# Attention with values stationary in two column groups, probabilities scaled on GpSimd, and partitions moved by SBUF transfers

## The reference

```
q, k, v: (2, 8, 768, 64), proj: (64, 6)
bucket(q), bucket(k): six sign bits of q @ proj and k @ proj
scores = where(bucket(q) == bucket(k), q @ k.T / 8, -1e9)
attn = exp(scores - rowmax); attn = attn / (rowsum + 1e-9)
x = attn @ v                                  -> (1536, 512)
h = x @ w_in (512, 2048); g = P(h) / Q(h);    x2 = g @ w_out
route: expert = argmax(x2 @ w_gate); out = gate * relu(x2 @ w1[e]) @ w2[e], 8 experts
```

## Time and profile before

| | us |
|---|---|
| median of 3 runs | 906.86 |
| lowest, highest | 903.77, 913.84 |
| the profiled execution | 908.51 |
| its span | 906.7 |
| busy PE / DVE / ACT / POOL | 853.0 / 761.4 / 598.5 / 365.1 |
| chain that ended last: PE, DVE, ACT | 72%, 15%, 5% |
| granted TensorE clock, mean | 0.98 |

### The profile page before, as it was taken

The page is one execution under the profiler, slowest core; times in us unless marked ns, Lnnn a source line. Parts: engine busy times, 40 slices in busy tenths (PEclk is TensorE's granted clock), DMA queues, the critical chain, the costliest instruction groups (busy, mean ns, idle before and its releaser), DMA issues.

```text
span 906.7 us, 17000 instructions
## 1 busy us (share of the span) xinstructions
PE 853.0 (94%) x5056; PEld 751.2 (83%) x5056; DVE 761.4 (84%) x1364; ACT 598.5 (66%) x1106; POOL 365.1 (40%) x321
## 2 busy tenths in 40 slices
PE   5999999999999998888999999999789999999996
PEld 3788989889898897777999998997678888888885
DVE  4789888888988759999877877876789999999992
ACT  1565666556566457567766776765279888998883
POOL 2553333534334406564222222222134666666542
PEclk7999999999999899999999999999989999999999
DMA  4111111211110101111000000002478111344950
GB/s 94 36 49 40 47 38 38 55 43 53 38 38 20 44 2 47 58 47 47 2 1 12 23 0 11 24 0 104 150 270 285 61 38 43 130 130 139 341 186 0
DMA packets 57472, 63.05 MB, mean 70 GB/s; under 512 B 29347, under 2 KB 39587, under 8 KB 57444
## 3 DMA queue, kind: packets, MB, share of 16 engines
q1 hardware_dynamic: 54404, 54.57, 19.2%
q0 software_dynamic: 3040, 8.13, 2.8%
HBM read 102.53 MB, written 8.13 MB: 122 GB/s over the span
## 4 chain that ended last, share of the span: by engine, by line
PE 72%; DVE 15%; ACT 5%; issue 4%; DMA 2%; POOL 1%; DVEq 0%; ACTq 0%; SPq 0%; POOLq 0%
PE ps_s L513 11%; PE ps_t L678 11%; PE ps_s L655 11%; PE ps_o L429 10%; PE ps_t L531 7%; PE ps_t L418 6%; PE ps_o L531 3%; PE ps_s L404 3%; PE ps_s L406 3%; DVE inv_b L1046 3%; DVE k_mask L909 2%; DVE row_max L923 2%; DVE num_b L1044 2%; PE ps_s L664 2%; PE ps_p L393 2%
## 5 line engine op out<-in xcount | busy, mean ns | idle before, releaser
L429 PEld LDWEIGHTS ps_o<-v_raw,probsT 128*128 128x128 f32 x1152 | 142.8, 194 | 5.7 <-issue 5.6
L1325 POOL TENSOR_TENSOR g_lo<-num_b,g_hi 128x384 fp32r<-128x384 f32 x64 | 65.3, 1020 | 190.2 <-ACT g_hi L793 113.4
L429 PE MATMUL ps_o<-v_raw,probsT 128*128 128x64 f32 x1152 | 141.5, 273 | 0.2 <-ACT x_pair L733 0.2
L1208 DVE TENSOR_TENSOR w_lo<-w_raw,w_hi 128x1024 fp32r<-128x1024 f32 x76 | 125.6, 1709 | 2.9 <-ACT w_hi L840 0.9
L719 ACT ACTIVATE probs<-ps_s,exp_bias,exp_scale 128x768 f32<-128x768 f32 x96 | 94.9, 989 | 44.5 <-DVE exp_bias L933 44.5
L923 DVE TENSOR_REDUCE row_max<-ps_s 128x1 f32<-128x768 f32 x96 | 91.1, 949 | 16.3 <-PE ps_s L406 16.3
L418 PE MATMUL ps_t<-ident,probs 128*128 128x128 f32 x576 | 82.4, 280 | 8.8 <-DVE probsT L938 6.6
L733 ACT ACTIVATE x_pair<-ps_o,row_inv 128x64 f32<-128x64 f32 x96 | 30.1, 314 | 88.5 <-PE ps_o L429 88.5
L513 PE MATMUL ps_s<-xT_hi,win_hi 128*128 (+1 forms) x256 | 88.0, 344 | 0.0
L513 PE MATMUL ps_s<-xT_hi,win_lo 128*128 (+1 forms) x256 | 86.2, 337 | 0.0
L418 PEld LDWEIGHTS ps_t<-ident,probs 128*128 128x128 f32 x576 | 66.1, 146 | 24.3 <-issue 20.5
(11 more groups left out here) (210 smaller groups left out, 2271.9 us busy)
## 6 DMA issues: line engine op xcount, KB each, us to landing
w_raw<-in_moe_w_dram SPq DMA_DIRECT2D x152, 512.0 KB
win_raw<-in_moe_w_in_dram SPq DMA_DIRECT2D x16, 256.0 KB, 2.8
x_sb<-in_moe_w_out_dram SPq DMA_DIRECT2D x16, 256.0 KB, 2.6
qk_raw<-in_q_dram SPq DMA_DIRECT2D x16, 192.0 KB, 3.1
qk_raw<-in_k_dram SPq DMA_DIRECT2D x16, 192.0 KB, 3.4
v_raw<-in_v_dram SPq DMA_DIRECT2D x16, 192.0 KB, 2.4
mlp_out_scratch<-x_sb SPq DMA_DIRECT2D x12, 256.0 KB, 2.0
out_dram<-y_sb,idx_scatter POOLq DMA_INDIRECT x19, 2.8
```

What stands on the lines that cost most here:

```text
L429: mm = pe.matmul(ps_o[:, 0:D], probsT[slot][:, t, :], v_raw[par][:, t, :], start=(t == 0), stop=(t == QT - 1))
L1208: dve.tensor_tensor(w1_lo[par][:, c, :], w1_raw[:, c, :], w1_hi[par][:, c, :].bitcast(F32), ALU.subtract).then_inc(w1_lo_made, 1)
```

## The change

On PE, `attend` now takes two tiles at once, every second step: v (64 columns) is stationary and the turned probabilities (128 columns) move. One tile's result goes to PSUM partitions 0 to 63, the other's to 64 to 127 (two column groups of the array). x so comes out turned, and `turn_x` is gone. The two halves of a hash go to two column groups as well; `hash_w` is 64 columns wide.

The probabilities are scaled before they are turned, by POOL (`normalise`); ACT's `norm` is gone. DVE makes the inverses of two tiles together. There are three buffers of probabilities and four of turned ones. PE turns a tile two steps after its exp and attends four steps after; scores are made two steps ahead.

High parts of q and k, masks and x go through staging tiles, and SP moves them to their places by transfers from SBUF to SBUF: four for the high parts, four for the masks, four for x, per head. One `mask_rows` per head replaces four. POOL's w_in split uses a one-input instruction. At the start q and k of both heads are turned before the first hash; at the end the first three `mlp_up` are put between the last steps, and the second stage waits for the transfers of x.

```diff
@@ SP
+            def place_hi(par):
+                hi = qkT_hi[:].bitcast(F32)
+                for target, rows, part in ((k_mask, slice(0, D), slice(D, P)), (q_mask, slice(0, D), slice(0, D)),
+                                           (k_cross, slice(0, D), slice(D, P)), (q_cross, slice(D, P), slice(0, D))):
+                    sp.dma_start(target[par][rows, :].bitcast(F32), hi[part, :]).then_inc(hi_in[par], 16)
+            def place_masks(par):
+                for hb in range(2):
+                    cols = slice(hb * HALF, (hb + 1) * HALF)
+                    for target, row in ((q_mask, HC * hb), (k_mask, HC * hb + ZK)):
+                        sp.dma_start(target[par][D:KR, cols].bitcast(F32),
+                                     mask_st[row:row + MR, :]).then_inc(mask_in[par], 16)
+            def place_x(i, par):
+                for parts, target in ((x_hi_st, xT_hi), (x_lo_st, xT_lo)):
...
+                    for g in range(2):
+                        sp.dma_start(blocks[:, where, g, :, :], parts[par][g * D:(g + 1) * D, :].bitcast(F32).rearrange(
+                            "p (o b n) -> p o b n", o=1, b=BLOCKS)).then_inc(x_out[par], 16)
+            def attention_head(i, par, first=False, more=True, more_qk=True):
+                m = 2 * i + par
+                if not (first and par == 0):
+                    if more or par == 0:
+                        hold(sp, masked, m + 2)
+                        hold(sp, scored, QT * m)
+                        place_masks(1 - par)
+                        hold(sp, attended, BLOCKS * m)
+                        load_v(m + 1, 1 - par)
+                    hold(sp, x_lo_made, START + m)
+                    place_x(i if par else i - 1, 1 - par)
+                if more:
+                    hold(sp, win_lo_made, m + 1)
+                    load_win(m + 2, par)
+                    if more_qk:
+                        hold(sp, qk_turned, 2 * m + 6)
+                        load_qk(m + 4, par)
+                    hold(sp, qk_hi_made, m + 3)
+                    hold(sp, scored, QT * (m + 1))
+                    place_hi(par)
@@ PE
+            def hash_qk(i, par):
+                pe.wait_ge(qk_copied, 4 * i + 2 * par + 2)
+                for hb in range(2):
+                    mm = pe.matmul(ps_p[HC * hb:HC * (hb + 1), 0:HALF], hash_w[:],
+                                   qkT[:, hb * HALF:(hb + 1) * HALF], start=True, stop=True)
             def scores(...)
+                    pe.wait_ge(mask_in[par], 64 * (i + 1))
+                    pe.wait_ge(hi_in[par], 64 * (i + 1))
+                    pe.wait_ge(qk_parts, 4 * i + 2 * par + 2)
+                if not first:
+                    pe.wait_ge(exped, STEPS * i + c - 1)
             def turn_probs(...)
-                pe.wait_ge(exped, n + 1)
+                pe.wait_ge(normed, n + 1)
+            def attend(i, c):
+                n, par, b = STEPS * i + c, c // QT, (c % QT) // 2
+                pe.wait_ge(pT_lo_half, n + 2)
+                pe.wait_ge(pT_hi_half, n + 2)
+                if b == 0:
+                    pe.wait_ge(v_in[par], 16 * (i + 1))
+                    pe.wait_ge(x_lo_made, START + 2 * i + par)
                 for t in range(QT):
-                    mm = pe.matmul(ps_o[:, 0:D], probsT[slot][:, t, :], v_raw[par][:, t, :],
-                                   start=(t == 0), stop=(t == QT - 1))
+                    for g in range(2):
+                        mm = pe.matmul(ps_o[g * D:(g + 1) * D, b * P:(b + 1) * P], v_raw[par][:, t, :],
+                                       probsT[(c + g) % 4][:, t, :], start=(t == 0), stop=(t == QT - 1))
+            def step(i, c):
+                if c % 2 == 0 and there(i, c - 4):
+                    attend(*at(i, c - 4))
+                if there(i, c - 2):
+                    turn_probs(*at(i, c - 2), first=isinstance(i, int) and STEPS * i + c == 2)
+                if there(i, c + 2):
+                    scores(*at(i, c + 2))
+                if there(i + 1, 0):
+                    if c % QT in (1, 3):
+                        turn_qk(i + 1, c // QT, c % QT // 2)
+                    if c % QT == 5:
+                        hash_qk(i + 1, c // QT)
@@ ACT
+            def step(i, c):
+                if there(i, c):
+                    exp_scores(i, c)
+                if c % QT in (2, 4) and there(i + 1, 0):
+                    copy_qk(i + 1, c // QT, c % QT // 2 - 1)
+                if c % QT == 3 and there(i, c - QT):
+                    x_hi(*((i, 0) if c >= QT else (i - 1, 1)))
+                if there(i, c - 2):
+                    copy_probs(*at(i, c - 2))
@@ DVE
+            def mask_rows(i, par, first=False):
...
+                dve.tensor_scalar(mask_st[:], ps_p[:, 0:HALF], hash_thr[:, 2:3], hash_thr[:, 3:4],
+                                  ALU.is_ge, ALU.mult).then_inc(masked, 1)
+            def step(i, c):
+                if there(i, c + 1):
+                    find_max(*at(i, c + 1))
+                    row_scale(*at(i, c + 1))
+                    row_bias(*at(i, c + 1))
+                if c % 2 == 1 and there(i, c):
+                    invert_sums(i, c)
+                if there(i, c - 2):
+                    copy_probs(*at(i, c - 2))
+                if c % QT == 0:
+                    if c == 0 and there(i, 0) and not (isinstance(i, int) and i == 0):
+                        mask_rows(i, 1)
+                    if c == QT and there(i + 1, 0):
+                        mask_rows(i + 1, 0)
+                if c % QT == 3 and there(i, c - QT):
+                    x_lo(*((i, 0) if c >= QT else (i - 1, 1)))
@@ POOL
+            def normalise(i, c):
+                slot = probs[c % 3]
+                if c % 2 == 0:
+                    pool.wait_ge(inverted, PAIR_TILES * i + c // 2 + 1)
+                pool.tensor_scalar(slot[:], slot[:], row_inv[:, c:c + 1], None, ALU.mult).then_inc(normed, 1)
+            def attention_pair(i, more):
+                for par in range(2):
+                    for j in range(QT):
+                        normalise(i, QT * par + j)
+                        if j == 1:
+                            split_win(i, par)
+                        if more and j == 3:
+                            hi_of_qk(i + 1, par)
+                            lo_of_q(i + 1, par)
+                        if more and j == 5:
+                            lo_of_k(i + 1, par, STEPS * i + QT * (par + 1))
@@ PE, between attention and the second stage
+            step(PAIRS, 0)
             pe.wait_ge(win_lo_made, PIECES)
...
             mlp_up(0, 0)
+            step(PAIRS, 1)
+            mlp_up(0, 1)
+            step(PAIRS, 2)
+            pe.wait_ge(exped, STEPS * PAIRS)
+            mlp_up(0, 2)
+            pe.wait_ge(x_lo_made, START + HEADS)
+            for par in range(2):
+                pe.wait_ge(x_out[par], 16 * START + 64 * PAIRS)
```

More of the change, by code:

```diff
@@ L482, in _ @@
             pe.wait_ge(ident_made, 2)
-            for hb in range(2):
-                turn_qk(0, 0, hb, first=True, bank=(ps_p, ps_t[0])[hb])
+            turn_qk(0, 0, 0)
+            turn_qk(0, 0, 1, bank=ps_t[0])
+            turn_qk(0, 1, 0, bank=ps_t[1])
+            turn_qk(0, 1, 1, bank=ps_s[0][:, 0, :])
+            pe.wait_ge(hash_made, 7)
+            hash_qk(0, 0)
             pe.wait_ge(consts_in, 64)
@@ L487, in _ @@
             pe.matmul(ps_o[:, 0:6], ones_row[:], ab_row[:, 0:6], start=True, stop=True).then_inc(coef_ps, 1)
[L488 to L504 removed]
+            pe.wait_ge(qk_copied, 4)
+            scores(0, 0, first=True)
+            scores(0, 1, first=True)
+            pe.wait_ge(masked, 1)
+            hash_qk(0, 1)
+            pe.wait_ge(coef_made, 2)
+            for c in range(STEPS):
+                step(0, c)
+            with pe.Fori(1, PAIRS - 1) as i:
+                for c in range(STEPS):
+                    step(i, c)
+            for c in range(STEPS):
+                step(PAIRS - 1, c)
             def mlp_up(g, f):
@@ L705, in _ @@
         def _(act):
-            for signal in (normed, logit_made, y_weighted):
+            for signal in (logit_made, y_weighted):
                 act.sem_inc(signal, START)
@@ L740, in step, with x_hi @@
-            def step(i, c, first=False, last=False):
-                n = STEPS * i + c
-                if not (last and c + 1 >= STEPS):
-                    exp_scores(n + 1, (c + 1) % STEPS)
-                copy_probs(n, c % 2)
-                if not (first and c == 0):
-                    norm(n - 1, (c - 1) % STEPS)
-                if c == 2 and not first:
-                    x_hi(i - 1, 1)
-                if c in (3, 4) and not last:
-                    copy_qk(i + 1, 0, c - 3)
-                if c in (8, 9) and not last:
-                    copy_qk(i + 1, 1, c - 8)
-                if c == 11:
-                    x_hi(i, 0)
+            def x_hi(i, par):
+                act.wait_ge(attended, BLOCKS * (2 * i + par + 1))
```

(24 more changed lines are left out.)

411 lines of the change are left out of this document (155 added, 256 removed).

## The result

The changed kernel takes **931.5 us** (median of 4 runs, 928.1 to 933.0) against 907.8 beside it (4 runs, 903.8 to 913.8): a ratio of 1.025 (95% interval 1.019 to 1.032). That is slower, though the interval leaves open whether by more than 2%. Forecast were 850 us and a range of 836 to 913. The profiled execution has a span of 929.3 us.

The account below looks back on a forecast made before the run. PE was taken as the bound, DVE close behind. First score 16, heads 249.6, -2.9, clock +5, latencies 2 put the last exp at about 270 instead of 331: -61, end +3.7; 908.5 - 57 - 1.6 = 850 us, range 836 to 913.

Parts of the forecast that it names:

- The scaling's price: POOL's scaling of one 128x768 tile of probabilities: 0.83 us taken, the lower of its bounds, the upper being 1.81.
- two small DVE steps at 0.16 us: Making the inverse on DVE, between bias and scaling: two steps of 0.16 us with 0.1 of gaps.
- Rival B: A new bound in attention, scaling at 1.81 us (898 us) or a lower PE clock (890 us); chance 0.14.
- The column groups: In attend on PE, both groups run at once: two tiles take 1.3 us plus 0.2 for entering and leaving.
- rival D: As C, and each passage between whole array and column groups costs 0.16 us, eight a head: 934 us; chance 0.11.
- C: Column groups in attend don't run together: 2.6 us for two tiles, head 19.6 us, 907 to 913 us; chance 0.16.
- Two tiles in 4.3 us: In attention, PE's own sum and the loop of waits each take 4.3 us for two tiles, 12.9 a head.
- ACT: no cost: ACT in attention loses its scaling and was busy for 27.81 of 45 us, so it costs nothing.
- The wait for x_lo: Between heads, PE's next attend waits until DVE has subtracted x_lo: 1.3 us a head, second turn included.
- Moves by DMA and the masks: SP's 12 more transfers a head cost 0, hidden by 2 to 3 us; landing 2.4 us, issuing 0.35 to 0.60.
- First score at 16: At the start, the second head's turns and the masks' transfer put the first score at 16 us instead of 14.46.
- The end, 19 us: From the last exp's start to the first down product: 19 us instead of 15.3, +3.7.

Follow-up runs that it names:

- Experiment 1: Changed kernel with POOL scaling by a constant 1.0 instead of the per-partition factor, probabilities left unscaled: 867.5 us.
- experiment 2: Changed kernel with DVE's two-column sum made as two one-column steps, scaling as in the changed kernel: 918.6 us.
- experiment 6: Changed kernel with POOL's scaling factor as a broadcast second tensor, the two-column sum left as it is: 870.7 us.
- experiment 3: Experiment 1 with attend's two loops exchanged, all passes of one column group ahead of the other's: 911.8 us.
- experiment 7: experiment 5 with the next tile's exp ahead of the copy of turned probabilities on ACT, and a fourth probability buffer: 922.7 us.
- experiment 9: Experiment 8 with exp ahead of the copy on ACT only in the steps that hold an attend: 870.0 us.
- Experiment 8: experiment 5 with the hash and its loads ahead of the second head's turns and loads at the start, as before the change: 867.7 us.
- experiment 5: Changed kernel with POOL's scaling factor as a broadcast second tensor and the sum made column by column: 872.4 us.
- experiment 4: Kernel before, with POOL's copy of qkT to qkT_hi multiplied by a column of ones, as pointer scalar or broadcast by head: 905.1 us.
- experiment 10: experiment 5 with DVE scaling the even tile of each two and POOL keeping the odd one: 971.2 us.

## Why the prediction was wrong

- **The scaling's price: the step that failed.** "I take 0.83, as one tensor comes in", between bounds of 0.83 and 1.81. It measured 2.20, outside both bounds. The row of 0.83 was the same shape with a *constant*; the change reads the factor from SBUF, one per partition, a form that POOL runs nowhere in the kernel before. The upper bound was a two-input pass over 64 partitions; nothing excluded a dearer form. So POOL, put down as no cost, sets the head. Six times 1.37 us make its 12.5 a head 20.7; that this meets the measured 20.76 is luck, as the 12.5 held 1 us too much for w_in and gaps, and 1.2 of the 20.76 is the sum's stall on top of POOL's own 19.6. The forecast's own sign for this was "scaling over 1 us (B)", and it came. Experiment 1 puts 64 us on the price, of which 13 come by way of the sum (experiment 2).
 The Trainium skill's page GPSIMD Engine Reference, Engine selection, calls a one-input operation roughly line-rate; the pass with a constant, 0.83, comes near that (by an estimate of one element a cycle at that page's 1.2 GHz, 0.64 us), the one with a pointer scalar, 2.20, does not. Its section Elementwise — side-by-side cycle accounting gives 2.6 cycles an element for two inputs, an estimate of 1.66 us for this shape at that page's 1.2 GHz; 1.47 was measured.
- **The loop's "two small DVE steps at 0.16 us".** Right for one column. The change made one step of two columns, which waits for POOL's two-input passes. Only with POOL late did this cost anything (experiments 2 and 6).
- **Rival B** named the mechanism and its place ("scaling costs 1.81, POOL 18.4 us a head", 898), at a chance of 0.14. With the head as measured it would have been 850 + 15 x (20.75 - 15.6) = 927, and with start and end as below 934, against 931.5.
- **The column groups: right.** 24 passes take 1.53 us, 1.5 was forecast, and experiment 3 shows that the alternation carries it. From an attend's start to the next transposes it is 1.46 us (experiment 1's timeline):
```profile
104.24 1.53 PE L487 MATMUL ps_o<-probsT,v_raw 128*64 128x128 f32 x24 [0.60 <-DVE x_lo_st L966]
...
105.70 0.64 PEld L474 LDWEIGHTS ps_t<-ident,probs 128*128 128x128 f32 x6 [0.17 <-issue]
```
 Leaving the groups does cost something: the first transpose starts 0.20 us behind the last pass of the attend, each time, where before, from attend to transpose, it was 0.11. That is 0.09 us a passage, where rival D had 0.16, and it lies in the 0.2 an attend that the forecast had. So 872, the forecast's time for the drain with groups in parallel, is met by the 871 of experiment 6 only by chance. With the groups in turn the head is C's (19.3 measured, 19.6 forecast), not D's.
- **Two tiles in 4.3 us: too little.** Experiment 1 has all that the forecast assumed. Its attends start 5.50, 5.28 and 5.77 us apart (at 104.24, 109.73, 115.01 and 120.78). From start to start the hash takes 0.70 of the first, a turn 0.33 of each of the others, and the wait for x_lo 0.6 of the last: 4.8 to 4.95 are left, 0.5 to 0.6 more, three times a head. Less the 0.4 that the forecast had for the mask, and less what the wait for x_lo came out shorter, that is a head of 16.5, not 15.6. "ACT: no cost" hid it: exp stands behind the copy that waits for the turn, and the odd step's scores wait for exp, 0.4 us three times a head (experiment 1's waits). But experiments 7 and 9 show that neither of two other orders gives it back; the waits move to exp for its bias and to the attend for the copies. So the order on ACT alone is not what sets it. Which member of the loop would have to be shortened is open.
- **The wait for x_lo: there, and a little too large.** The forecast's 1.3 held the second turn as well. Once POOL is on time it is 0.33 for the turn and 0.6 of waiting; after, with POOL late, PE waited for it 14 times, 17.7 us in all.
- **Moves by DMA and the masks: right** in the heads. No score waits for a transfer there, though a mask's transfer takes SP 0.7 to 0.9 us to issue instead of 0.35 to 0.60, and the high parts take 3.9 to 4.4 us to land, not 2.4. In the first head, one turn waits 3.3 us for a load of k that SP issues behind the masks' transfers; before, no turn in the heads waited so.
- **First score at 16: it came at 19.7.** I counted the second head's turns on PE and not its loads. These stand in SP's queue ahead of the constants of the hash. So DVE prepares these late, beside POOL's two-input passes over q_cross (8.57 to 10.38 us) and k_cross (10.46 to 12.26), which costs two tiny steps 3 us:
```profile
8.61 1.81 DVE L996 TENSOR_SCALAR hash_w<-proj 64x6 f32<-64x6 f32 x1
...
10.77 1.50 DVE L1003 TENSOR_TENSOR hash_thr<-hash_thr 64x1 f32<-64x1 f32 x1
```
 Experiment 8 gives 4.6 us back by order alone.
- **The end, 19 us: it took 21.8,** and still 21.0 with the fast scaling (last exp at 288.77, first down product at 309.76 in experiment 1). The sum of that stretch was 2 us short in itself.
- **Does it close?** 850, +15 for the head (16.6 for 15.6), +3.6 for the start, +2 for the end: 871, where experiments 5 and 6 measure 872.4 and 870.7. From the first down product on 560 us were forecast, and 557.9 came.

## What to carry to other kernels

Before work moves to an engine, find a row of the very form of instruction, operand kinds included: constant, pointer scalar and broadcast tensor gave 0.83, 2.20 and 1.47 us for one shape on POOL. Where no such row exists the upper bound is open, and an engine's sum per period should be asked at which price it becomes the bound (here, an estimate, by the forecast's own sums, at 0.83 + (15.6 - 12.5) / 6 = 1.35 us). If an engine turns out late, look at what the form costs before rearranging the order: one line gave 61 us, three attempts at order gave +50, +2 and -5.

## What the runs showed of the hardware

- **POOL, 128x768 f32:** 832 ns by a constant, 1467 by a broadcast column, 2203 by a pointer scalar; over 8 to 96 instances the extremes are 17 ns apart at most (after, experiments 1, 4, 5). Only beside DVE's pass of the same shape did the broadcast form take up to 1893 (experiment 10).
- **DVE beside POOL's two-input passes:** 128x2 and 64x6 steps with one source, and a two-source 64x1, that start inside such a pass do not end before it (up to 1.8 us); a one-source 128x768 pass went from 0.62 to 1.92 us, or POOL's from 1.47 to 1.84; 128x1 sums do not wait (142 to 153 ns).
- **Column groups in f32:** 24 passes of 64 stationary and 128 moving columns take 1.53 us alternating by product and 2.46 us in turn; from the last of them to a transpose with the whole array it is 0.20 us, from an attend with the whole array 0.11.
- **The granted clock** stayed at 1.00 in windows of 45 us with PE busy for 33.51 (after) and 34.90 (experiment 7), and was 0.92 in experiment 7's next one. There, 0.63 and 0.52 in 2 us each followed 2 us in which PE was busy for 0.14.
